# One tile in four of the bias network moved to GpSimd, and the first head's q, k and bias rows prepared in the bias stage

## The reference

```
q, k, v: [4, 8, 576, 64]       (batch, head, position, width)
x[i, j]   = log1p(|i - j|) / log1p(max(i, 1))
bias      = relu(x * w1 + b1) @ w2          hidden 32, one output per head
attn      = softmax(q k^T / 8 + bias)       over j
x         = attn v                          -> [2304, 512]
x         = (s * relu(x w_in)^2 + b) w_out  512 -> 2048 -> 512
h         = x w_in2;  out = (h - tanh(h)) w_out2
```

## Time and profile before

| | us |
|---|---|
| median of 3 runs | 1247.45 |
| lowest, highest | 1245.78, 1251.20 |
| the profiled execution | 1251.22 |
| its span (first to last instruction) | 1249.4 |
| bias stage, first tile to last mirrored copy | 6.07 to 71.02 |
| first product of block 2 | 75.65 |

### The profile page before, as it was taken

One profiled execution on the slowest core, in us unless ns is written; L12 is line 12 of the kernel. 1 busy time (PEld: TensorE's weight loads), 2 busy tenths in 40 slices (PEclk: granted clock), 3 DMA queues, 4 the chain that ended last, 5 costly groups with the idle time before them and its releaser, 6 DMA issues.

```text
span 1249.4 us, 17895 instructions
## 1 busy us (share of the span) xinstructions
PE 1158.2 (93%) x6274; PEld 1023.6 (82%) x6274; DVE 729.3 (58%) x1456; ACT 749.8 (60%) x1426; POOL 564.8 (45%) x443
## 2 busy tenths in 40 slices
PE   4647776799999999999999999999999999999999
PEld 1136665689999999999999999999998888899998
DVE  5846666777557765865776586567626145162350
ACT  8945445567567656756766576567547355374452
POOL 0023233345454545545455445454344545555454
PEclk9867677699999999999999999999999999999999
DMA  3563333434444453454445544544233323333332
GB/s 134 193 240 101 118 116 95 128 108 146 154 145 152 139 193 129 152 172 147 147 133 173 157 138 158 159 140 135 83 119 106 111 93 101 131 119 115 105 101 80
DMA packets 66777, 167.66 MB, mean 134 GB/s; under 512 B 8032, under 2 KB 14848, under 8 KB 66688
## 3 DMA queue, kind: packets, MB, share of 16 engines
q1 hardware_dynamic: 66400, 166.44, 41.7%
q10 hardware_dynamic: 288, 0.07, 0.0%
HBM read 150.87 MB, written 15.61 MB: 133 GB/s over the span
## 4 chain that ended last, share of the span: by engine, by line
PE 85%; ACT 6%; DVE 4%; issue 3%; DMA 1%; SPq 0%; DVEq 0%; ACTq 0%
PE ps_f L602 21%; PE ps_f L604 21%; PE ps_f L603 21%; PE ps_t L429 7%; PE ps_o L394 4%; PE ps_o L396 3%; PE ps_s L410 3%; PE ps_s L411 3%; ACT hid L242 3%; DVE ptl L504 1%; ACT stage L260 1%; ACT pth L437 1%; DVE p_t L497 1%; ACT p_t L444 1%; PE ps_f L429 1%
## 5 line engine op out<-in xcount | busy, mean ns | idle before, releaser
L559 POOL TENSOR_TENSOR wl<-w_raw,wh 128x512 fp32r<-128x512 f32 x320 | 426.5, 1338 | 493.8 <-ACT wh L552 493.4
L602 PE MATMUL ps_f<-xh,wh 128*128 128x464 f32 (+1 forms) x640 | 242.4, 379 | 1.8 <-DVE xl L578 1.8
L602 PE MATMUL ps_f<-gh,wh 128*128 128x464 f32 (+1 forms) x640 | 243.5, 380 | 0.0
L604 PE MATMUL ps_f<-xh,wl 128*128 128x464 f32 (+1 forms) x640 | 238.6, 373 | 0.0
L603 PE MATMUL ps_f<-xl,wh 128*128 128x464 f32 (+1 forms) x640 | 238.0, 372 | 0.0
L603 PE MATMUL ps_f<-gl,wh 128*128 128x464 f32 (+1 forms) x640 | 237.4, 371 | 0.0
L604 PE MATMUL ps_f<-gh,wl 128*128 128x464 f32 (+1 forms) x640 | 237.3, 371 | 0.0
L552 ACT ACTIVATE wh<-w_raw 128x512 fp32r<-128x512 f32 x320 | 197.8, 623 | 41.0 <-PE ps_f L604 41.0
L437 ACT ACTIVATE pth<-ps_t 128x576 fp32r<-128x576 f32 (+1 forms) x144 | 93.8, 651 | 190.9 <-PE ps_t L429 190.5
L504 DVE TENSOR_TENSOR ptl<-ps_t,pth 128x576 fp32r<-128x576 f32 (+1 forms) x144 | 108.9, 756 | 121.7 <-ACT pth L437 121.4
L497 DVE CUSTOM_DVE_ANT_0 p_t<-ps_s,bias_t 128x576 f32<-128x576 f32 x160 | 120.2, 751 | 39.6 <-PE ps_s L411 37.7
(11 more groups left out here) (72 smaller groups left out, 1639.6 us busy)
## 6 DMA issues: line engine op xcount, KB each, us to landing
w_raw<-in_w_in SPq DMA_DIRECT2D x80, 512.0 KB, 3.7
w_raw<-in_w_out SPq DMA_DIRECT2D x80, 512.0 KB, 3.7
bias_t<-bias_flat SPq DMA_DIRECT2D x128, 288.0 KB, 2.8
bias_flat<-stage SPq DMA_DIRECT2D x36, 295.5 KB, 2.1
q_raw<-in_qt SPq DMA_DIRECT2D x32, 288.0 KB, 3.1
k_raw<-in_kt SPq DMA_DIRECT2D x32, 288.0 KB, 4.5
v_raw<-in_vt SPq DMA_DIRECT2D x32, 160.0 KB, 2.9
bias_t<-bias_flat SPq DMA_DIRECT2D x32, 144.0 KB, 3.1
```

The source lines that it names most:

```text
L559: pool.tensor_tensor(wl[:, b % RING, :, :], w_raw[:, b // 2 % RAW, b % 2, :, :], wh[:, b % RING, :, :].bitcast(F32), ALU.subtract).then_in ...
L602: pe.matmul(acc, hi, rhs_h[:, k0 + kk, 0:T], start=(first and kk == 0), stop=False)
L604: mm = pe.matmul(acc, lo, rhs_h[:, k0 + kk, 0:T], start=False, stop=(last and kk == 3))
```

## The change

`SHIFTED = 3` is added beside `VEC = 2`: DVE keeps tiles 0 and 1 of each pack, POOL computes tile 2 with DVE's formula, and ACT keeps tile 3. PE waits for a third semaphore, `hid_pool`. `const` now covers the partitions of three tiles. In pack 2 (`LATE`) ACT rounds q and k of head 0, behind its copy of that pack; in pack 4 POOL forms the two remainders. SP issues the bias loads of head 0 within block 1: the load of rows 128 t to 128 t + 127 comes after the store of pack 9, 17, 25 and 33, and waits until the stores of the packs 0 to 7, 0 to 15, 0 to 23 and 0 to 31 have landed; the last load (64 rows) comes after the last store and waits for all of them, still in block 1. The same instructions are gone from the start of block 2; the helper functions have moved up in the file.

```diff
+SHIFTED = 3
+LATE = 2
@@ SP, block 1
+            def load_bias(sp, t):
+                packs = min(PACKS, (t + 1) * P // ROW)
+                for i in range(RES_BUFS):
+                    sp.wait_ge(stage_stored[i], packs // RES_BUFS * DMA)
+                if t == NT - 1:
+                    sp.wait_ge(bias_clear, 1)
+                sp_bias(sp, 0, t)
...
                     sp.dma_start(rows, stage[:, pack % RES_BUFS, 0:back + ahead])\
                         .then_inc(stage_stored[pack % RES_BUFS], DMA)
+                    t, late = divmod(pack - LATE + 1, P // ROW)
+                    if t and not late:
+                        load_bias(sp, t - 1)
+                load_bias(sp, NT - 1)
@@ ACT, block 1
-                    for at in range(VEC, PACK):
+                    for at in range(SHIFTED, PACK):
...
                     mm.then_inc(ahead_done, 1)
+                    if pack == LATE:
+                        act.wait_ge(q_clear, 2)
+                        act.wait_ge(lower_done, 2)
+                        act_round_q(act, 0)
+                        act_round_k(act, 0)
@@ POOL, block 1
+                pool.wait_ge(table_done, 3)
+                for pack in range(PACKS):
+                    need(pool, hid_used, pack - HIDS + 1)
+                    n = reach(pack)
+                    for at in range(VEC, SHIFTED):
+                        step = pack * PACK + at
+                        mm = pool.tensor_scalar(hid[:, pack % HIDS, at, 0:n], psi_t[:, 0:n],
+                                                slope[:, step:step + 1], nb1_c[:, 0:1], ALU.mult, ALU.max)
+                    mm.then_inc(hid_pool, 1)
+                    if pack == 2 * LATE:
+                        pool_low_q(pool, 0)
+                        pool_low_k(pool, 0)
@@ PE, block 1
                     pe.wait_ge(hid_act, pack + 1)
+                    pe.wait_ge(hid_pool, pack + 1)
@@ start of block 2
-            for i in range(RES_BUFS):                                  (SP)
-                sp.wait_ge(stage_stored[i], PACKS // RES_BUFS * DMA)
-            sp.wait_ge(bias_clear, 1)
-            for t in range(NT):
-                sp_bias(sp, 0, t)
...
-            pool_low_q(pool, 0)                                        (POOL)
-            pool_low_k(pool, 0)
...
-            act.wait_ge(q_clear, 2)                                    (ACT)
-            act.wait_ge(lower_done, 2)
-            act_round_q(act, 0)
-            act_round_k(act, 0)
```

More of the change, by code:

```diff
@@ L106, in build @@
         hid_act = sem("hid_act")
+        hid_pool = sem("hid_pool")
         no_const = sem("no_const")
@@ L172, in load_v, with act_round_q, act_round_k, pool_low_q @@
             sp.dma_start(v_raw[:].rearrange("p t d -> p (t d)"), vt[n]).then_inc(v_loaded, DMA)
+        def act_round_q(act, n):
+            act.wait_ge(qk_loaded, (n + 1) * 2 * DMA)
+            need(act, s_done, (n - 1) * NT)
+            act.activation(q2[:, n % 2, 0:S], q_raw[:], ACT.Copy, scale=lower[:, 0:1]).then_inc(q_hi_done, 1)
+        def act_round_k(act, n):
+            act.activation(k2h[:, n % 2, :], k_raw[:], ACT.Copy).then_inc(k_hi_done, 1)
+        def pool_low_q(pool, n):
+            pool.wait_ge(q_hi_done, n + 1)
+            both = q2[:, n % 2, 0:S]
+            pool.tensor_tensor(both, q_raw[:], both.bitcast(F32), ALU.subtract).then_inc(q_lo_done, 1)
+        def pool_low_k(pool, n):
+            pool.wait_ge(k_hi_done, n + 1)
+            need(pool, s_done, (n - 1) * NT)
+            pool.tensor_tensor(k2l[:, n % 2, :], k_raw[:], k2h[:, n % 2, :].bitcast(F32), ALU.subtract)\
+                .then_inc(k_lo_done, 1)
+        def sp_bias(sp, n, t):
+            R = ROWS[t]
+            rows = bias_skew[P * t:P * t + R, bass.ds(n % H * PITCH + (S - 1), S)]
+            sp.dma_start(bias_t[0:R, t, :], rows).then_inc(bias_loaded[t], DMA)
         with ExitStack() as bctx:
@@ L230, in _ @@
                 act.dma_start(lam_c[:], lam).then_inc(psi_loaded, DMA)
-                shifted = slice(0, VEC * G * H)
+                shifted = slice(0, SHIFTED * G * H)
                 act.wait_ge(const_done, 1)
@@ L272, in _ @@
                                    pattern=[[-1, P]], channel_multiplier=1).then_inc(ident_done, 1)
+                pool.wait_ge(table_done, 3)
[10 more added lines that the diff above has]
+                        pool_low_k(pool, 0)
             @block.vector
             def _(dve):
-                dve.memset(const[VEC * G * H:P, :], 0.0).then_inc(no_const, 1)
+                dve.memset(const[SHIFTED * G * H:P, :], 0.0).then_inc(no_const, 1)
                 dve.memset(lower[0:D, :], 0.0).then_inc(lower_done, 1)
@@ L456, in act_step @@
                 act.activation(vhl[:, n % 2, :, 0:D], v_raw[:], ACT.Copy).then_inc(v_hi_done, 1)
[L458 to L475, removed]
         def pool_step(pool, n, t):
@@ L531, in sp_step @@
                 load_v(sp, n + 1)
[L533 to L536, removed]
         def sp_weights(sp, pair):
@@ L680, in _ @@
         def _(sp):
-            for i in range(RES_BUFS):
-                sp.wait_ge(stage_stored[i], PACKS // RES_BUFS * DMA)
-            sp.wait_ge(bias_clear, 1)
-            for t in range(NT):
-                sp_bias(sp, 0, t)
             load_qk(sp, 1)
@@ L706, in _ @@
         def _(pool):
-            pool_low_q(pool, 0)
-            pool_low_k(pool, 0)
             for n, t in STEPS_AT[:FIRST]:
@@ L722, in _ @@
             act.wait_ge(sb_loaded, DMA)
-            act.wait_ge(q_clear, 2)
-            act.wait_ge(lower_done, 2)
-            act_round_q(act, 0)
-            act_round_k(act, 0)
             for n, t in STEPS_AT[:FIRST]:
```

## The result

The changed kernel is slower: 1258.11 us median of 11 runs against 1248.54, ratio 1.0077 with a 95% interval from 1.0047 to 1.0106, that is 6 to 13 us. The prediction was 1237 with a range up to 1248, so the sign was wrong too. The profiled execution took 1255.1, span 1253.3.

A forecast was written before the change was run, and what follows sets the result against it. ACT was taken to bound the bias stage early and DVE late, DVE and POOL after the change. Stage 8.0, seam 1.5 and k of head 1 1.0 sum to 10.5 us off the 1247.45 median: 1237, range 1231 to 1241, to 1248 with rivals.

The forecast's parts named there:

- What bounds now: Bias stage before the change: ACT sets the pace early at 1.79 us a pack, DVE at the end at 1.78.
- DVE's list: Bias stage: 45 us of DVE work after taking tails off 49.4; with 3 us fill and drain, 48 if unhindered.
- POOL's tile: Tile 2 of each pack in the bias stage: 0.70 us at 440 columns, with bounds of 0.45 and 1.12.
- the other side: Rival, chance 0.12: POOL's tile costs 1.12 us and stops DVE throughout; stage 72, kernel 1252; loss from about 0.99 a tile.
- It is no bound by itself: POOL in the bias stage: 25 us for 36 tiles plus 2.8 for the remainders, so not limiting alone.
- The sentences on the Trainium skill's figures: POOL's tile at about line-rate for one input: 0.59 us at 440 columns, stage 53 us, kernel 1233.
- The lock: Bias stage: POOL's instruction stops DVE's SBUF tiles but not its PSUM copy; fully against each other 59.1 us, taken as 57.
- The remainders in POOL's list: POOL's remainders of q and k, moved into the stage, stop DVE's tiles for up to 1.4 us each, once.
- The seam: From stage end to PE's start in block 2: 3.1 us instead of 4.67, a gain of 1.5.
- q and k of head 1: Loads at block 2's start: k lands 4.7 us after issue, ACT waits 2.1 instead of 3.2; 1.0 gained.
- The transfers: Stores and loads in the stage: 210 GB/s against 194; SP's new waits cost nothing, at most 0.5 us four times.
- The sum: Whole kernel: stage 8.0, seam 1.5 and k of head 1 1.0 make 10.5 us gained.

The follow-up runs named there:

- POOL cheap: The changed kernel with POOL's tile cut to 100 columns in every pack, the rest filled by a clear at the start; ratio 0.992 to the kernel before.
- the runs with a faster stage: Changed kernel with POOL's tile cut to 100 columns (ratio 0.992); kernel with three DVE tiles in packs below 13, none on POOL, preparation in the stage (0.9954).
- the preparation alone: Against the kernel before, only roundings, remainders and bias loads of head 0 moved into the stage; ACT keeps tiles 2 and 3; ratio 0.9985.
- three tiles on DVE early, roundings at pack 34: Three DVE tiles in packs below 13, none on POOL, roundings behind pack 34, last bias load moved to block 2; ratio 0.9908 to the kernel before.

## Why the prediction was wrong

- **What bounds now**: right. ACT gave the pace early, DVE late, and with POOL cheap the stage fell to 56.7 us; DVE was busy 48.3 of it, and all the time from 38 us on.
- **DVE's list**: 45 us was too low. I took the tails of about 70 instructions off the 49.4, but the windows count a time in which two instructions overlap only once: in the kernel before the durations of DVE's 112 instructions add up to 55.8 us, and the window has 49.4. With POOL cheap the list was 48.3, so the floor of 48 for the stage was one for DVE's list alone.
- **POOL's tile**: the step that failed. "I take 0.21 + 440 x 1.1 ns = 0.70 us", with 1.12 as the bound from above, both from neighbouring rows. It measured 1.83 at 440 columns, 2.6 times the value and 1.6 times the bound. The bound rested on the thought that two tensors from SBUF must cost more than one tensor and scalars; the measurement has it the other way round (2.28, or 1.73 with one operation, against 1.15 for the broadcast product and 1.40 for the subtraction at 576). No row of the kernel before showed the form, so the range should have been open upwards. The rival "the other side" named the mechanism, a long loop on POOL, and put its turning point at 0.99 us; its price and its 12% were too low.
- **"It is no bound by itself"** followed from the price. By the measured one POOL's list is 36 x 1.83 + 2.8 = 69 us, over the old stage's 65 before any contention. The trace has 72.2, and the stage 74.9. DVE's list no longer set the pace in any part of the stage: PE waited for POOL in 33 places.
- **The sentences on the Trainium skill's figures** (GPSIMD Engine Reference, Engine selection: one input about line-rate) pointed to 0.59 us. The runs contradict that for this operation, 1.83 by the measured line and 1.73 at 576 columns even with one scalar; the measurement decides. The section's general advice, that elementwise work is VectorE's, would have served better here.
- **The lock**: wrong in form, small in effect. "DVE stood still as long as POOL's instruction ran" fits the one subtraction read in the earlier trace rows, not this operation: DVE completed whole tiles within it and lost 0.8 of 2.8 us. The sum of the excess on DVE's tiles in the changed kernel, 40.2 - 32.9 = 7.3 us, lies in the 6 to 10 that I named, but by luck, since POOL's tiles were 2.8 times as long as assumed; DVE was not the bound. What I had left out is that POOL is stretched too, and POOL was the bound: 69.3 us against 36 x 1.83 = 65.9 undisturbed, an estimated 3.4 us of the loss. The rule of the Trainium skill (SBUF, Who interferes with whom), an exclusive lock for the whole instruction, does not agree with the two DVE tiles of 0.57 us that started and ended within POOL's 2.82. POOL free beside the copy from PSUM: right.
- **The remainders in POOL's list**: priced as a stop of DVE, up to 1.4 us each. They cost 3.2 us because POOL was the bound.
- **The seam**: 1.0 gained for 1.5 predicted, with 3.7 for 3.1 from the last copy. The bias load is issued 2.3 after the copy, as taken, but the engines start only 1.2 to 1.5 later, where I had 0.32 + 0.5. In the runs with a faster stage it is issued 3.2 to 3.7 after the copy, PE starts 4.6 to 5.1 after it (4.67 before), and the gain is gone.
- **q and k of head 1**: 2.4 gained for 1.0. I put k's landing at 4.7 us after its issue, and it landed 3.4 after (84.81 to 88.26); with the preparation alone it took 4.5. What makes that difference isn't shown.
- **The transfers**: the 210 GB/s were set against 194, which is one window of the stage; over the whole stage the kernel before has 169, and the run with the cut tile 205. ACT waited 1.7 us there for stage tiles to be stored, where I had put such waits at nothing.
- **The sum**: 10.5 predicted; about 10 measured once POOL's tile cost 0.89 us. One term decided the sign, but the agreement of the rest is luck: in the run with the cut tile the stops of DVE were 0.9 us and not 9, its list without them 47.4 and not 45, its idle time 8.4 and not 3; the seam gave 1.9 less than I took and k 1.4 more.

## What to carry to other kernels

Before a tile is moved to an engine, measure that form of instruction on that engine by itself; a row of a neighbouring form is no bound, not even from above. Then compare its whole time with the pace of the loop, not its share with the idle time of the engine: here one tile in four at three times DVE's price became the new bound. And when a total comes out as predicted, look whether its parts do. Work that has a wait ahead of it (loads, roundings, stores) may be moved over a barrier only with a look at what the barrier then waits for; the last store's landing belongs to the one engine that needs it.

## What the runs showed of the hardware

- On GpSimd, a product and maximum with two scalars takes 0.37 us and 3.33 ns a column (128 partitions, float32), with one operation 1.73 us at 576; the product with a broadcast tensor 1.15, at the same width.
- A DVE instruction from SBUF to SBUF with scalars (0.57 us at 576) and this GpSimd instruction share only parts of their time: four DVE instructions started during one of 2.82 us, two of them took 0.57.
- In these GpSimd instructions against DVE's at 576 columns both are stretched (GpSimd 2.28 to 2.82). In the changed kernel DVE's tiles of up to 368 columns were not stretched, those of 480 were, from 0.52 to 0.85.
- The whole time goes with the mean granted clock of the run: eight executions of one kernel (three tiles on DVE early, roundings at pack 34) ran from 1225.85 us at 0.976 to 1242.45 at 0.950, 16.6 us apart, more than the change cost. The profiles differ in the first heads (0.70, 0.73 and 0.89 in 85 to 250 us in three of them). Stages are to be compared by marks ahead of that stretch, whole times by many runs.
